# Pair 0 of an attention kernel started from k, q in two halves, constants asked for by GpSimd, zeros multiplied ahead of k

## The chip, the core and the metric

One NeuronCore of a Trainium2 chip runs the whole program. TensorE (PE) multiplies, VectorE (DVE), ScalarE (ACT) and GpSimd (POOL) work element by element, and SyncE (SP) only asks for DMA transfers; ScalarE asks for some too. Each engine takes its instructions in the order written and waits on semaphores. The metric is the device time of one execution in microseconds.

## What is computed

Attention in which a query sees only the keys of its own bucket (six sign bits of a random projection), for 16 heads of 768 rows and 64 columns, and two feed-forward layers behind it:

```python
q_bits = (np.einsum('bhsd,dk->bhsk', q, proj) > 0)
k_bits = (np.einsum('bhsd,dk->bhsk', k, proj) > 0)
mask = q_bucket[:, :, :, None] == k_bucket[:, :, None, :]
scores = scale * np.matmul(q, k.transpose(0, 1, 3, 2))
scores = np.where(mask, scores, -1000000000.0)
attn = np.exp(scores - np.max(scores, axis=-1, keepdims=True))
attn = attn / (np.sum(attn, axis=-1, keepdims=True) + 1e-09)
x = np.matmul(attn, v)
# layer 1: h = x @ w_in, g = P(h) / (Q(h) + 1e-06), x = g @ w_out
# layer 2: h = x @ w_in, g = h - np.tanh(h), out = g @ w_out
```

## The kernel before

Two heads make a pair; there are eight pairs, then the two layers. A pair has 12 tiles of 128 query rows, six of head e=0 and six of head e=1. For each tile TensorE makes scores of 128x768 in one of two PSUM buffers `slot` (`pe_scores`), VectorE takes the row minimum (`dve_rowmin`, L571; scores are negated), ScalarE the exponential E (`act_exp`, L459), TensorE transposes E in two halves into `turn_ps` (`pe_tile`, L379), ScalarE rounds each half to `pt_hi` (L520), VectorE subtracts to get `pt_lo` (L613), and TensorE multiplies both with v (`pe_pv`). Scores are made `AHEAD` = 3 tiles early; `pe_att`, `act_att` and `dve_att` write out the order of each engine tile by tile (n = 0 to 11).

Products keep float32 accuracy by splitting an operand in a rounded high part and the rest. For scores the operands are `opA[e][x]` and `opB[e][x]` (qA, kA, qB, kB in the trace; x = 0 is q, 1 is k). Half of the partitions of opA are "hot" rows, which carry the bucket: q and k are transposed (`turned`, q_t and k_t), multiplied with the projection `proj_bd` (dots), compared with zero (`bits`), the bits multiplied with `pats`, and the result compared with `counts`. A score of two different buckets is then pushed away by 2^120.

While a pair runs, q and k of the next are turned in between its tiles (`pe_turn`, `act_turned`, L266 and L405), and GpSimd splits them. Pair 0 has nobody ahead of it. Its preparation is `pe_first`, `act_first`, `dve_first` and `pool_first`: q is loaded by SP, k by ScalarE, each in two transfers (one for each head). TensorE transposes q in two halves (L296), then k; ScalarE copies q_t and splits q, VectorE copies k_t; four dots give all bits in one tile of 128 partitions, one VectorE instruction makes `bits` (L556), four products the hot rows (L311), which VectorE (q, L563) and ScalarE (k, L431) write. GpSimd makes the low parts of head 0 and then all parts of head 1. Then follow three scores, three row minima (`dve_first` ends with them), and two exponentials (`act_first`). In the first tiles of pair 0 ScalarE also copies the turned q and k of pair 1 (four L405), which wait for GpSimd's count `t_op1`, since `turned` is overwritten.

SP's queue holds, in this order: q, four pieces of the projection, `pats`, `counts`, v, q and k of pair 1 (each waits for the transposes that free its buffer), the coefficients of the layers, six weight tiles, and then what the pairs need.

Of the kernel before, what the change touches and what calls it, by code (L numbers as in the profile page):

```python
# [30 lines left out]
def build(nc, q, k, v, proj, w_in1, w_out1, coef_a, coef_b, w_in2, w_out2,  # L31
# [42 lines left out]
            for names in ADDED_BY.values() for name in names}  # L74
    loads = {name: top.enter_context(nc.semaphore("s_" + name))
             for name in ["ident", "consts", "coefs", "ready", "coef", "proj", "q", "k", "v", "out", "ops0", "ops1",
                          "scale_out0", "scale_out1", "scale_in0", "scale_in1", "shift0", "shift1", "pool_here", "sync_here"]
             + ["t_turn", "t_q", "t_k", "t_dots", "t_bits", "t_hot", "t_hot_q", "t_hot_k",
                "t_hi_q", "t_hi_k", "t_hi_kb", "t_lo", "t_op1"]
# [11 lines left out]
    with top:  # L91
# [70 lines left out]
        first_bank = [[aux_ps, pv_ps], turn_ps]  # L162
        att.close()
# [124 lines left out]

        def pe_first(eng):

            eng.wait_ge(loads["ident"], 16)
            for x in range(2):
                eng.wait_ge(loads["qk"[x]], 32)
                for h in range(2):
                    for c in range(G):
                        mm = eng.transpose(first_bank[x][h][:, c * P:(c + 1) * P],  # L296
                                           nat[x][:, h * G + c, :, :], ident[:, :])
                    mm.then_inc(loads["t_turn"], 1)
            eng.wait_ge(loads["coef"], 1)
            for x in range(2):  # L300
                eng.wait_ge(loads[("t_q", "t_k")[x]], 2)
                for h in range(2):
                    o = (2 * x + h) * KB
                    mm = eng.matmul(slot[0][o:o + KB, 0, 0:HALF], proj_bd[:, x, :],
                                    turned[x][:, h * HALF:(h + 1) * HALF], start=True, stop=True)
            mm.then_inc(loads["t_dots"], 1)
            eng.wait_ge(loads["consts"], 32)
            eng.wait_ge(loads["t_bits"], 1)
            for h in range(2):
                for x in range(2):  # L310
                    eng.matmul(first_bank[x][h][:, 0:HALF], pats[:, 2 * x + h, :], bits[:, :],  # L311
                               start=True, stop=True).then_inc(loads["t_hot"], 1)
# [31 lines left out]
        def pe_att(eng, p, first=False, prepare=True, turn=True, last=False):  # L344
            for n in range(TILES - G * last):
                pe_tile(eng, p, n)
                if first and n < 2:
                    pe_turn(eng, 1, n, 0)
# [8 lines left out]
                if first and n + AHEAD == T:  # L357
                    eng.wait_ge(loads["t_op1"], 6)
# [49 lines left out]

        def act_first(eng):
            hs = [slice(0, HALF), slice(HALF, S)]  # L410
            for h in range(2):
                eng.wait_ge(loads["t_turn"], h + 1)
                eng.activation(turned[0][:, hs[h]], first_bank[0][h][:, 0:HALF], ACT.Copy,
                               scale=-1.0 / float(D) ** 0.5).then_inc(loads["t_q"], 1)
            eng.wait_ge(loads["proj"], 64)
            eng.activation(proj_bd[:, 0, :], proj_bd[:, 0, :], ACT.Copy, scale=-1.0
                           ).then_inc(loads["coef"], 1)
            eng.wait_ge(loads["t_q"], 2)
            eng.activation(opA[0][0][0:D, :], turned[0][0:D, :], ACT.Copy
                           ).then_inc(loads["t_hi_q"], 1)  # L420
            eng.activation(opB[0][0][D:2 * D, :], turned[0][0:D, :], ACT.Copy
                           ).then_inc(loads["t_hi_q"], 1)
            eng.wait_ge(loads["t_k"], 2)
            eng.activation(opA[0][1][0:D, :], turned[1][0:D, :], ACT.Copy
                           ).then_inc(loads["t_hi_k"], 1)
            eng.wait_ge(loads["consts"], 32)
            for e in range(2):
                o = D - e * D
                for h in range(2):
                    eng.wait_ge(loads["t_hot"], 2 * h + 2)  # L430
                    eng.activation(opA[e][1][o:o + D, hs[h]], first_bank[1][h][o:o + D, 0:HALF],  # L431
                                   ACT.Relu, bias=counts[o:o + D, 1:2]
                                   ).then_inc(loads["t_hot_k"], 1)
            eng.wait_ge(loads["ready"], 3)
# [69 lines left out]
        def act_att(eng, p, first=False, prepare=True, turn=True, last=False):  # L504
            for n in range(TILES):
# [17 lines left out]
                if first and n < 2:  # L523
                    eng.wait_ge(loads["t_op1"], 3 * n + 3)
# [21 lines left out]

        def dve_first(eng):
            hs = [slice(0, HALF), slice(HALF, S)]
            for h in range(2):
                eng.wait_ge(loads["t_turn"], h + 3)  # L550
                eng.tensor_copy(turned[1][:, hs[h]], first_bank[1][h][:, 0:HALF]
                                ).then_inc(loads["t_k"], 1)
            eng.wait_ge(loads["t_k"], 2)
            eng.tensor_copy(opB[0][1][0:D, :], turned[1][0:D, :]).then_inc(loads["t_hi_kb"], 1)
# [802 lines left out]
```

## Time and profile before

| | us |
|---|---|
| three runs | 767.23, 767.30, 768.35 (median 767.3) |
| the profiled execution | 767.21 |
| its span, first to last instruction | 765.0 |
| TensorE busy | 751.2 (98%) |
| VectorE, ScalarE, GpSimd busy | 536.6, 478.4, 155.5 |

A row of the timeline tells the start and length of an instruction, or of several of one kind in a row (x2: both together, with what lay between them), and in brackets how long the engine stood idle ahead of it and what ended that. Transfers are listed by the issuing queue (SPq, ACTq); the length there is that of the issue, and landing is told apart. The ends of matmuls are modelled.

### The profile page before, as it was taken

To read this page: it belongs to the slowest core of one execution; us is meant where nothing else is said; L and a number is where in the kernel's file an instruction comes from. 1 tells how busy PE (TensorE), PEld (TensorE's weight loads), DVE (VectorE), ACT (ScalarE), POOL (GpSimd) and SP (SyncE) were. 2 spreads that over 40 slices of the span, in tenths; PEclk is the share of its full clock that TensorE was granted. 3 is DMA by queue.
4 is the path that set the end of the run, shared out by engine and by line. 5 is a ranking of instruction groups with operands and counts; after the bars stand their busy time and mean duration, and the time that the engine had idled before them with its cause. 6 is when DMAs were issued, how large, how long until landed. Compare 5 with 4: busy or idle time off the path is not lost.

```text
span 765.0 us, 11965 instructions
## 1 busy us (share of the span) xinstructions
PE 751.2 (98%) x3840; PEld 642.1 (84%) x3840; DVE 536.6 (70%) x856; ACT 478.4 (63%) x940; POOL 155.5 (20%) x133
## 2 busy tenths in 40 slices
PE   5999999999999999999999999999999999999998
PEld 3899999999998877888888888888888888888886
DVE  4888988988997999999988898955442322233222
ACT  5989988988997877788766876755332222222221
POOL 5784665566566000000000000000000000000000
PEclk9999999999999999999999999999999999999999
DMA  7678778877753410000000233330000100001001
GB/s 196 145 170 204 172 178 185 188 177 179 164 130 99 146 51 32 1 1 1 0 1 15 55 95 99 93 87 1 0 1 1 56 0 1 0 1 56 0 1 56
DMA packets 65243, 58.11 MB, mean 76 GB/s; under 512 B 31792, under 2 KB 50480, under 8 KB 65200
## 3 DMA queue, kind: packets, MB, share of 16 engines
q1 hardware_dynamic: 63488, 57.09, 29.6%
q10 hardware_dynamic: 1712, 0.46, 0.3%
q8 instruction: 25, 0.41, 0.2%
q14 instruction: 18, 0.15, 0.1%
HBM read 29.57 MB, written 3.19 MB: 43 GB/s over the span
## 4 chain that ended last, share of the span: by engine, by line
PE 84%; DVE 12%; issue 2%; ACT 1%; ACTq 0%; DVEq 0%
PE acc L822 28%; PE h_ps L793 27%; PE slot L253 9%; PE turn_ps L379 8%; PE pv_ps L337 4%; PE pv_ps L339 4%; DVE sqr L967 2%; DVE pol L988 2%; DVE pol L999 2%; DVE pol L974 1%; DVE pol L980 1%; PE aux_ps L266 1%; DVE sqr L991 1%; DVE wout_lo L1028 1%; DVE g_lo L1012 1%
## 5 line engine op out<-in xcount | busy, mean ns | idle before, releaser
L793 PE MATMUL h_ps<-x_hi,win_lo 128*128 128x512 f32 x384 | 149.7, 390 | 0.0
L793 PE MATMUL h_ps<-x_lo,win_hi 128*128 128x512 f32 x384 | 149.4, 389 | 0.0
L793 PE MATMUL h_ps<-x_hi,win_hi 128*128 128x512 f32 x384 | 149.4, 389 | 0.0
L843 ACT ACTIVATE g_hi<-pol 128x512 fp32r<-128x512 f32 x96 | 60.8, 633 | 125.6 <-PE acc L822 100.4
L1012 DVE TENSOR_TENSOR g_lo<-pol,g_hi 128x512 fp32r<-128x512 f32 x96 | 66.0, 687 | 97.9 <-ACT g_hi L843 97.7
L613 DVE TENSOR_TENSOR pt_lo<-turn_ps,pt_hi 128x384 fp32r<-128x384 f32 x192 | 97.8, 550 | 18.8 <-ACT pt_hi L520 17.3
L520 ACT ACTIVATE pt_hi<-turn_ps 128x384 fp32r<-128x384 f32 x192 | 84.1, 494 | 15.2 <-PE turn_ps L379 13.8
L571 DVE TENSOR_REDUCE row_min<-slot 128x1 f32<-128x768 f32 x96 | 90.4, 942 | 1.5 <-PE slot L253 1.5
L459 ACT ACTIVATE E<-slot,row_min 128x768 f32<-128x768 f32 x96 | 88.1, 918 | 4.2 <-DVE row_min L571 2.6
L793 PEld LDWEIGHTS h_ps<-x_lo,win_hi 128*128 128x128 f32 x384 | 72.1, 188 | 15.0
L793 PEld LDWEIGHTS h_ps<-x_hi,win_hi 128*128 128x128 f32 x384 | 72.1, 188 | 15.0
L793 PEld LDWEIGHTS h_ps<-x_hi,win_lo 128*128 128x128 f32 x384 | 72.0, 188 | 14.7
L1006 DVE TENSOR_TENSOR pol<-h_ps,mag 128x512 f32<-128x512 f32 x48 | 33.1, 691 | 67.7 <-ACT mag L866 67.2
L379 PE MATMUL turn_ps<-ident,E 128*128 128x128 f32 x576 | 79.6, 273 | 0.0
L866 ACT ACTIVATE mag<-h_ps 128x512 f32<-128x512 f32 x48 | 28.7, 598 | 78.4 <-PE h_ps L793 75.2
L822 PE MATMUL acc<-g_hi,wout_lo 128*128 128x512 f32 x192 | 75.2, 392 | 1.0 <-DVE g_lo L1012 0.8
L822 PE MATMUL acc<-g_hi,wout_hi 128*128 128x512 f32 x192 | 74.7, 389 | 0.0
L822 PE MATMUL acc<-g_lo,wout_hi 128*128 128x512 f32 x192 | 74.7, 389 | 0.0
L822 PE MATMUL acc<-wout_lo,g_hi 128*128 128x512 f32 x192 | 74.7, 389 | 0.0
L822 PE MATMUL acc<-wout_hi,g_hi 128*128 128x512 f32 x192 | 74.7, 389 | 0.0
L822 PE MATMUL acc<-wout_hi,g_lo 128*128 128x512 f32 x192 | 74.7, 389 | 0.0
L379 PEld LDWEIGHTS turn_ps<-ident,E 128*128 128x128 f32 x576 | 68.0, 140 | 5.3 <-DVE pt_lo L613 1.9
(119 smaller groups left out, 1375.6 us busy)
## 6 DMA issues: line engine op xcount, KB each, us to landing
win_raw<-in_moe_w_in SPq DMA_DIRECT2D x32, 256.0 KB, 3.2
wout_raw<-in_moe_w_out SPq DMA_DIRECT2D x32, 256.0 KB, 3.0
q_nat<-in_q SPq DMA_DIRECT2D x16, 192.0 KB, 3.3
v_nat<-in_v SPq DMA_DIRECT2D x8, 384.0 KB, 3.4
scale<-softmax_scale SPq DMA_DIRECT2D x16, 192.0 KB, 3.2
k_nat<-in_k SPq DMA_DIRECT2D x14, 192.0 KB, 3.6
qA<-q_hi SPq DMA_DIRECT2D x14, 192.0 KB, 2.6
qB<-q_hi SPq DMA_DIRECT2D x14, 192.0 KB, 3.0
```

The costliest lines, as they stand in the source:

```text
L253: mm = eng.matmul(slot[m % 2][:, h, 0:HALF], ops[e][0][:, i * P:(i + 1) * P], ops[e][1][:, h * HALF:(h + 1) * HALF], start=first, stop=not ...
L337: eng.matmul(pv_ps[:, 0:HALF], vv, pt_hi[:, c % 2, kt, :], start=kt == 0, stop=False)
L379: mm = eng.transpose(turn_ps[h][:, c3 * P:(c3 + 1) * P], E[:, n % RING, kt * P:(kt + 1) * P], ident[:, :])
L459: eng.activation(halves(E[:, m % RING, :]), slot[m % 2][:, :, 0:HALF], ACT.Exp, bias=row_min[:, m % RING:m % RING + 1], scale=-1.0, accum_ ...
L520: eng.activation(pt_hi[:, c % 2, k0:k0 + T // 2, i * P:(i + 1) * P], turn_ps[h][:, 0:HALF].rearrange("r (k n) -> r k n", n=P), ACT.Copy).t ...
L571: eng.tensor_reduce(row_min[:, m % RING:m % RING + 1], slot[m % 2][:, :, 0:HALF], AX.XY, ALU.min).then_inc(sems["rowmin"], 1)
L613: eng.tensor_tensor(pt_lo[dst], turn_ps[h][:, 0:HALF].rearrange("r (k n) -> r k n", n=P), pt_hi[dst].bitcast(F32), ALU.subtract).then_inc( ...
L793: mm = eng.matmul(h_ps[t % 4][:, :], w[:, ws], columns(x, kt, c), start=kt + n == 0, stop=kt == KT - 1 and n == 2)
L822: mm = eng.matmul(acc[i][:, :], l, r if layer else r[:, :], start=j + n == 0, stop=j == J - 1 and n == 2)
L843: eng.activation(g_hi[:, t % TEMPS, :], pol[:, t % TEMPS, :], ACT.Copy).then_inc(mlp_sems["g_hi"], 1)
L1006: eng.tensor_tensor(pol[:, t % TEMPS, :], h_ps[t % 4][:, :], mag[:, t % 2, :], ALU.subtract).then_inc(mlp_sems["g"], 1)
L1012: eng.tensor_tensor(g_lo[:, b, :], pol[:, b, :], g_hi[:, b, :].bitcast(F32), ALU.subtract).then_inc(mlp_sems["g_lo"], 1)
```

## The change

In pair 0's preparation, and nowhere else:

- **Loads.** SP asks for k of one head, then for q in four pieces (two halves of the rows by two heads); ScalarE asks for the identity and k of the other head. GpSimd asks for `pats`, two pieces of the projection (four before) and `counts`, which SP did.
- **TensorE.** It multiplies zeros (a part of E's last buffer, set by VectorE) ten times, transposes k, then the first half of q. The products of bits and patterns take 32 partitions each. The second half of q is transposed behind k's patterns. Three and four more zero products stand ahead of the first and second scores. The third scores come behind the transposes of tile 0.
- **ScalarE and VectorE.** Each copies one half of k_t. ScalarE makes the projection for q as the negative of that for k, ahead of its copy. Bits are made in three pieces, the low part of q's first half by VectorE (`qB<-q_t,qA`), that of the second half by GpSimd. The row minimum of the third tile is taken behind pt_lo of tile 0.
- **GpSimd.** The casts and subtractions are reordered, k first.
- SP loads q of pair 1 after the transposes of q's second half (`t_turn` 4), k of pair 1 after those of k.

```diff
@@ pe_first
+            eng.wait_ge(loads["ready"], 1)
+            pe_busy(eng, 10)
             eng.wait_ge(loads["ident"], 16)
+            for h in range(2):
+                pe_first_turn(eng, 1, h)
+            pe_first_turn(eng, 0, 0)
+            eng.wait_ge(loads["t_k"], 2)
             eng.wait_ge(loads["coef"], 1)
+            for h in range(2):
+                mm = pe_first_dots(eng, 1, h, slot[1][:, 0, :])
             mm.then_inc(loads["t_dots"], 1)
+            eng.wait_ge(loads["t_q"], 1)
+            pe_first_dots(eng, 0, 0, slot[1][:, 0, :]).then_inc(loads["t_dots"], 1)
...
@@ act_first
+            eng.wait_ge(loads["proj"], 32)
+            eng.activation(proj_bd[:, 0, :], proj_bd[:, 1, :], ACT.Copy, scale=-1.0
+                           ).then_inc(loads["coef"], 1)
+            eng.wait_ge(loads["t_turn"], 2)
+            eng.activation(turned[1][:, HALF:S], first_bank[1][1][:, 0:HALF], ACT.Copy
+                           ).then_inc(loads["t_k"], 1)
+            act_first_q(eng, 0)
             for h in range(2):
+                act_first_hot(eng, 0, h)
+            act_first_q(eng, 1)
+            act_first_hot(eng, 1, 1)
...
@@ dve_first
+            eng.tensor_copy(opA[0][1][0:D, :], turned[1][0:D, :]).then_inc(loads["t_hi_k"], 1)
+            dve_first_bits(eng, slice(2 * KB, 4 * KB), slot[1][:, 0, :], 1)
+            eng.wait_ge(loads["t_hi_q"], 1)
+            eng.tensor_tensor(opB[0][0][0:D, 0:HALF], turned[0][0:D, 0:HALF],
+                              opA[0][0][0:D, 0:HALF].bitcast(F32), ALU.subtract
+                              ).then_inc(loads["t_lo_q"], 1)
+            dve_first_bits(eng, slice(0, KB), slot[1][:, 0, :], 2)
+            dve_first_hot(eng, 0, 0)
...
@@ dve_att
+                if first and n == 0:
+                    dve_rowmin(eng, 0, 2)
...
@@ SP
-                for e in range(2):
-                    eng.dma_start(nat[0][:, :, e, :], q_d[0, :, e]).then_inc(loads["q"], 16)
+                eng.dma_start(nat[1][:, :, 0, :], k_d[0, :, 0]).then_inc(loads["k"], 16)
+                for h in range(2):
+                    tiles = slice(h * G, (h + 1) * G)
+                    for e in range(2):
+                        eng.dma_start(nat[0][:, tiles, e, :], q_d[0, :, e, tiles]
+                                      ).then_inc(loads[("t_q0", "q")[h]], 16)
...
@@ gpsimd
+                eng.dma_start(pats[:, :, :], patterns).then_inc(loads["consts"], 16)
+                eng.wait_ge(loads["ready"], 2)
+                for e in range(2):
+                    eng.dma_start(proj_bd[e * D:(e + 1) * D, 1, e * NB:(e + 1) * NB], proj
+                                  ).then_inc(loads["proj"], 16)
+                eng.dma_start(counts[:, :], bit_counts).then_inc(loads["consts"], 16)
```

VectorE's queue in the preparation, from its copy of k_t to the last hot rows, before (kB0 is opB of head 0; the semaphores it waits for stand in brackets):

```order
L551 COPY k_t<-turn_ps0 128x384 [waits s_t_turn]
L551 COPY k_t<-turn_ps1 128x384 [waits s_t_turn]
L554 CAST kB0<-k_t 64x768 [waits s_t_k]
L556 TENSOR_SCALAR bits<-slot0 128x384 [waits s_t_dots]
L563 TENSOR_SCALAR qA0<-aux_ps,counts 64x384 [waits s_t_hot,s_consts]
L563 TENSOR_SCALAR qA0<-pv_ps,counts 64x384 [waits s_t_hot]
L563 TENSOR_SCALAR qA1<-aux_ps,counts 64x384 [waits s_t_hot]
L563 TENSOR_SCALAR qA1<-pv_ps,counts 64x384 [waits s_t_hot]
```

and after:

```order
L613 COPY k_t<-turn_ps0 128x384 [waits s_t_turn]
L616 CAST kA0<-k_t 64x768 [waits s_t_k]
L599 TENSOR_SCALAR bits<-slot1 64x384 [waits s_t_dots]
L619 TENSOR_TENSOR qB0<-q_t,qA0 64x384 [waits s_t_hi_q]
L599 TENSOR_SCALAR bits<-slot1 32x384 [waits s_t_dots]
L606 TENSOR_SCALAR qA0<-aux_ps,counts 64x384 [waits s_t_hot,s_consts]
L626 TENSOR_SCALAR kA1<-turn_ps0,counts 64x384 [waits s_t_hot]
```

The bits come in pieces, a subtraction of q (L619) stands between the first two, and a hot part of k (L626) is VectorE's now.

The same queue from the first row minimum to that of the fourth tile, before:

```order
L571 TENSOR_REDUCE row_min<-slot0 128x1 [waits s_scores0]
L571 TENSOR_REDUCE row_min<-slot1 128x1 [waits s_scores1]
L571 TENSOR_REDUCE row_min<-slot0 128x1 [waits s_scores0]
L613 TENSOR_TENSOR pt_lo<-turn_ps0,pt_hi 128x3x128 [waits s_pt_hi]
L613 TENSOR_TENSOR pt_lo<-turn_ps1,pt_hi 128x3x128 [waits s_pt_hi]
L571 TENSOR_REDUCE row_min<-slot1 128x1 [waits s_scores1]
```

and after:

```order
L637 TENSOR_REDUCE row_min<-slot0 128x1 [waits s_scores0]
L606 TENSOR_SCALAR qA1<-aux_ps,counts 64x384 [waits s_t_hot,s_consts]
L599 TENSOR_SCALAR bits<-pv_ps 32x384 [waits s_t_dots]
L637 TENSOR_REDUCE row_min<-slot1 128x1 [waits s_scores1]
L606 TENSOR_SCALAR qA0<-pv_ps,counts 64x384 [waits s_t_hot,s_consts]
L606 TENSOR_SCALAR qA1<-pv_ps,counts 64x384 [waits s_t_hot,s_consts]
L679 TENSOR_TENSOR pt_lo<-turn_ps0,pt_hi 128x3x128 [waits s_pt_hi]
L679 TENSOR_TENSOR pt_lo<-turn_ps1,pt_hi 128x3x128 [waits s_pt_hi]
L637 TENSOR_REDUCE row_min<-slot0 128x1 [waits s_scores0]
L637 TENSOR_REDUCE row_min<-slot1 128x1 [waits s_scores1]
```

Two instructions stand between the first and second row minimum, and the third one (slot0) has moved behind the two pt_lo.

GpSimd's queue at its start, before:

```order
L650 TENSOR_TENSOR qB0<-q_t,qA0 64x768 [waits s_t_hi_q]
L650 TENSOR_TENSOR kB0<-k_t,kA0 64x768 [waits s_t_hi_k,s_t_lo]
L660 CAST qA1<-q_t 64x768 [waits s_t_q,s_t_lo]
L662 CAST qB1<-q_t 64x768 [waits s_t_op1]
L664 TENSOR_TENSOR qB1<-q_t,qA1 64x768 [waits s_t_op1]
L660 CAST kA1<-k_t 64x768 [waits s_t_k,s_t_op1]
```

and after:

```order
L1390 DMA pats<-in_patterns 128x512
L1393 DMA proj_bd<-in_proj 64x6 [waits s_ready]
L1393 DMA proj_bd<-in_proj 64x6
L1395 DMA counts<-in_bit_counts 128x2
L727 CAST kB0<-k_t 64x768 [waits s_t_k]
L729 ISA
L729 TENSOR_TENSOR kB0<-k_t,kB0 64x768 [waits s_t_hi_kb]
L719 CAST kA1<-k_t 64x768 [waits s_t_lo]
```

Four transfers stand ahead, and k's parts of head 0 come before all of q's.

## Rows read from the trace of the kernel before

**Rows 1.** The page's first line.

```profile
span 765.0 us, 11965 instructions
```

**Rows 2.** Busy time by stretch: length, engines in order, clock, DMA share, GB/s.

```profile
5.00:10.00 5.00, 4.35 (x20) 2.62 (x20) 1.78 (x3) 3.40 (x6) 1.42 (x1) 1.00 0.96 217
...
25.00:60.00 35.00, 35.00 (x240) 32.78 (x239) 31.05 (x55) 31.43 (x75) 24.50 (x25) 1.00 0.74 169
```

**Rows 3.** Chain of waits, 8 to 26 us: start, length, what.

```profile
18.96 1.01 ACT E L459 x2
...
22.84 0.85 PE aux_ps L275 x8
```

**Rows 4.** Timeline of the issuing queues, 0 to 8 us.

```profile
0.74 1.38 SPq L1203 DMA_DIRECT2D q_nat<-in_q  x2
2.31 2.43 SPq L1210 DMA_DIRECT2D proj_bd<-in_proj  x4
...
1.66 1.44 ACTq L1279 DMA_DIRECT2D k_nat<-in_k  x2
```

**Rows 5.** DMA issues, 0 to 30 us: count, KB each, us to landing.

```profile
proj_bd<-in_proj SPq DMA_DIRECT2D x4, 1.5 KB, 3.8
```

**Rows 6.** Timeline of TensorE, 0 to 26 us.

```profile
5.42 0.88 PE L296 MATMUL aux_ps<-ident,q_nat 128*128 128x128 f32 x3 [5.42 <-DMA q_nat<-in_q]
...
7.16 1.54 PE L296 MATMUL turn_ps<-ident,k_nat 128*128 128x128 f32 x6 [0.23 <-DMA k_nat<-in_k]
...
11.42 0.32 PE L311 MATMUL aux_ps<-bits,pats 128*128 128x384 bf16 x1 [1.23 <-DVE bits L556]
...
13.38 0.59 PE L253 MATMUL slot<-kA,qA 128*128 128x384 f32 x2 [1.15 <-ACT kA L431]
...
17.31 0.82 PE L379 MATMUL turn_ps<-ident,E 128*128 128x128 f32 x6
```

**Rows 7.** Timeline of VectorE, 0 to 26 us.

```profile
9.34 1.47 DVE L554 CAST kB<-k_t 64x768 fp32r<-64x768 f32 x1
10.73 0.54 DVE L556 TENSOR_SCALAR bits<-slot 128x384 bf16<-128x384 f32 x1
11.86 0.62 DVE L563 TENSOR_SCALAR qA<-aux_ps,counts 64x384 fp32r<-64x384 f32 x1 [0.58 <-PE aux_ps L311]
12.40 0.62 DVE L563 TENSOR_SCALAR qA<-pv_ps,counts 64x384 fp32r<-64x384 f32 x1
...
14.35 1.82 DVE L571 TENSOR_REDUCE row_min<-slot 128x1 f32<-128x768 f32 x2 [0.16 <-PE slot L253]
...
18.38 1.01 DVE L613 TENSOR_TENSOR pt_lo<-turn_ps,pt_hi 128x384 fp32r<-128x384 f32 x2
```

**Rows 8.** Timeline of ScalarE, 0 to 26 us.

```profile
6.97 0.49 ACT L413 ACTIVATE q_t<-pv_ps 128x384 f32<-128x384 f32 x1
...
15.39 0.90 ACT L459 ACTIVATE E<-slot,row_min 128x768 f32<-128x768 f32 x1 [1.27 <-issue]
...
16.29 0.89 ACT L459 ACTIVATE E<-slot,row_min 128x768 f32<-128x768 f32 x1
...
17.16 0.20 ACT L438 ACTIVATE cb_abs<-cb 128x2 f32<-128x2 f32 x1
17.83 0.87 ACT L520 ACTIVATE pt_hi<-turn_ps 128x384 fp32r<-128x384 f32 x2 [0.47 <-PE turn_ps L379]
```

**Rows 9.** Timeline of GpSimd, 0 to 26 us.

```profile
8.58 1.82 POOL L650 TENSOR_TENSOR qB<-q_t,qA 64x768 fp32r<-64x768 f32 x1 [8.12 <-ACT qA L419]
...
12.54 0.82 POOL L660 CAST qA<-q_t 64x768 fp32r<-64x768 f32 x1
```

**Rows 10.** Timeline of VectorE and GpSimd near the end of the pairs.

```profile
242.32 1.54 DVE L967 SCALAR_TENSOR_TENSOR sqr<-sqr,cb_abs,mag 128x512 f32<-128x512 f32 x1
...
247.91 0.75 DVE L967 SCALAR_TENSOR_TENSOR sqr<-sqr,cb_abs,mag 128x512 f32<-128x512 f32 x1
...
242.01 1.30 POOL L755 TENSOR_TENSOR win_lo<-win_raw,win_hi 128x512 fp32r<-128x512 f32 x1
```

More of the change, by code:

```diff
@@ L162, in build @@
         first_bank = [[aux_ps, pv_ps], turn_ps]
+        zeros = E[:, RING - 1, 0:HALF // 2].bitcast(BF16)
         att.close()
@@ L287, in pe_hot, with pe_busy, pe_first_turn @@
                        start=True, stop=True).then_inc(sems["aux"], 1)
+        def pe_busy(eng, n):
+            for _ in range(n):
+                eng.matmul(slot[1][:, 1, 0:HALF], zeros[:, 0:P], zeros, start=True, stop=True)
+        def pe_first_turn(eng, x, h):
+            eng.wait_ge(loads[("t_q0", "q", "k", "k")[2 * x + h]], 32)
+            for c in range(G):
+                mm = eng.transpose(first_bank[x][h][:, c * P:(c + 1) * P],
+                                   nat[x][:, h * G + c, :, :], ident[:, :])
+            mm.then_inc(loads["t_turn"], 1)
@@ new lines, in pe_first_dots, with pe_first_hot @@
+        def pe_first_dots(eng, x, h, bank):
+            o = (2 * x + h) * KB
+            return eng.matmul(bank[o:o + KB, 0:HALF], proj_bd[:, x, :],
+                              turned[x][:, h * HALF:(h + 1) * HALF], start=True, stop=True)
+        def pe_first_hot(eng, x, h):
+            rows = slice((2 * x + h) * KB, (2 * x + h + 1) * KB)
+            eng.matmul(first_bank[x][h][:, 0:HALF], pats[rows, 2 * x + h, :], bits[rows, :],
+                       start=True, stop=True).then_inc(loads["t_hot"], 1)
@@ L309, in pe_first @@
             for h in range(2):
-                for x in range(2):
-                    eng.matmul(first_bank[x][h][:, 0:HALF], pats[:, 2 * x + h, :], bits[:, :],
-                               start=True, stop=True).then_inc(loads["t_hot"], 1)
+                pe_first_hot(eng, 1, h)
+            pe_first_turn(eng, 0, 1)
+            eng.wait_ge(loads["t_bits"], 2)
+            pe_first_hot(eng, 0, 0)
+            pe_busy(eng, 3)
             eng.wait_ge(loads["t_hi_q"], 2)
@@ L356, in pe_att @@
                     pe_dots(eng, p + 2)
-                if first and n + AHEAD == T:
-                    eng.wait_ge(loads["t_op1"], 6)
+                if first:
+                    pe_first_operands(eng, n)
                 if n + AHEAD < TILES or not last:
@@ new lines, in dve_first_bits, with dve_first_hot @@
+        def dve_first_bits(eng, rows, bank, n):
+            eng.wait_ge(loads["t_dots"], n)
+            eng.tensor_scalar(bits[rows, :], bank[rows, 0:HALF], 0.0, None, ALU.is_gt
+                              ).then_inc(loads["t_bits"], 1)
+        def dve_first_hot(eng, e, h):
+            o = D - e * D
+            eng.wait_ge(loads["consts"], 32)
+            eng.wait_ge(loads["t_hot"], h + 3)
+            eng.tensor_scalar(opA[e][0][o:o + D, h * HALF:(h + 1) * HALF],
+                              first_bank[0][h][o:o + D, 0:HALF],
+                              counts[o:o + D, 0:1], BIG, ALU.is_lt, ALU.mult
+                              ).then_inc(loads["t_hot_q"], 1)
@@ L618, in dve_att @@
                     dve_scale(eng, p, n // T)
+                if first and n == 0:
+                    dve_rowmin(eng, 0, 2)
                 if last and n == TILES - 3:
@@ L1089, in load_qk @@
                     if is_zero(b - 1):
[L1090 removed]
+                        eng.wait_ge(loads["t_turn"], 4 - 2 * x)
                     else:
@@ L1277, in _ @@
                 eng.dma_start(ident[:, :], identity).then_inc(loads["ident"], 16)
-                for e in range(2):
-                    eng.dma_start(nat[1][:, :, e, :], k_d[0, :, e]).then_inc(loads["k"], 16)
+                eng.dma_start(nat[1][:, :, 1, :], k_d[0, :, 1]).then_inc(loads["k"], 16)
                 eng.preload_act_table_set("natural_log_exp_and_others")
@@ L1292, in _ @@
                 begin(eng, "dve")
+                eng.memset(zeros, 0.0).then_inc(loads["ready"], 1)
                 eng.memset(proj_bd[:, :, :], 0.0).then_inc(loads["ready"], 1)
@@ L1302, in _ @@
                 eng.wait_ge(loads["coefs"], 32)
-                eng.wait_ge(loads["ready"], 2)
+                eng.wait_ge(loads["ready"], 3)
                 dve_att(eng, PAIRS - 1, prepare=False, turn=False, last=True)
```

172 lines of the change are left out of this document (82 added, 90 removed).

## The prediction

> **What bounds the kernel now.** I read the page first, then the busy time by stretch, then the chain of waits, then the first 25 us engine by engine. The span is 765.0 us [rows 1]. From 25 us on TensorE has work all the time: 35.00 of 35.00 us in the stretch 25 to 60 [rows 2], and nothing behind 25 us is touched by the diff. So the change is worth what it moves the point where that regime begins, one for one. The chain of waits shows what sets this point: after the first tiles of pair 0 it runs through ScalarE (E at 18.96, then the copies of q_t and k_t that also turn pair 1) and gets to TensorE at 22.84 [rows 3]. ScalarE's pieces in between follow each other. The number to follow is therefore the start of the third exponential, E of tile 2, at 18.96; I call it E2. Ahead of it stand the first scores at 13.38 (S0) and the first transposes of E at 17.31 [rows 6].
>
> **When k is there.** Let K be the start of the k transposes, now 7.16. Behind q's start at 5.42 TensorE waits for DMA, and 192+64+192 KB have landed (768 rows of 64 floats are 192 KB); at 7.16 all 832 KB [rows 4 to 6]. That is 384 KB in 1.74 us, 221 KB/us. With k asked for first, one half of it from each queue, 192+64+96+192 = 544 KB stand before k's end if transfers are served in the order asked for: K = 5.42 + 96/221 = 5.85. Ends: 5.42, if the first q quarter yields, and 7.16, if the order does not matter. If the patterns (128 KB), now asked for early by GpSimd, go ahead of k too, K is 6.4. I take 5.85, nearest to the two rows it is interpolated from.
>
> **Zeros.** Ten multiplications keep TensorE working from about 1.5. Now six transposes take 1.54 us at 7.16, and six of the same size 0.82 at 17.31 [rows 6]: the slower of the two clock levels (1.2 and 2.4 GHz) by the rate, though the granted clock of that stretch reads 1.00 [rows 2]. I count the k transposes at the fast rate. If the zeros don't raise it, two groups of three and the dot products add about 0.7 us.
>
> **From K to the first scores, new order.** Three transposes reach a reader after 0.52 (17.31 to 17.83), the next three 0.33 later; the copy of 0.49 on ScalarE [rows 8] makes k_t whole at K+1.4. Then GpSimd casts to kB (0.82) and VectorE casts to kA at the same moment. They exclude each other: VectorE's cast of 64x768 at 9.34 took 1.47 us and ended at 10.81, 0.41 behind the end of GpSimd's operation (8.58+1.82 = 10.40) [rows 7, 9]. So GpSimd's low part of k starts at K+1.4+0.82+0.41+0.07 = K+2.7 and ends at K+4.5. Bits of k (0.54), the k patterns and ScalarE's casts all fit beside it. But VectorE's next instruction, the low part of q's first half, reads two operands in SBUF, and such a one waits too: the operation of 242.32 took 1.54 us, with GpSimd busy from 242.01 to 243.31, where its like takes 0.75 at 247.91 [rows 10]. It ended 0.55 behind GpSimd; for 384 columns I take 0.45. VectorE is free at K+4.95. Queued behind it are q's bits (0.54, to K+5.5), the pattern product (0.15+0.44, as from the end of bits at 11.27 over 11.42 to 11.86 [rows 6, 7]), the hot rows (0.62, to K+6.7), and the way to the scores (0.3, as 13.02 to 13.38). S0 = K+7.0 = 12.85, against 13.38: 0.5 us gained out of the 1.3 that k comes earlier. Halving q shortens ScalarE's and VectorE's pieces, but the path now goes through GpSimd.
>
> The Trainium skill (SBUF — State Buffer, Who interferes with whom) states this as a rule: a VectorE instruction with two SBUF inputs and a GpSimd one that reads SBUF lock each other out. It names tensor_tensor, the form used here, where my rows have another form. By its opposite, no lock, the sum would be the fourth rival's below.
>
> **From the first scores to E2.** Now it is 18.96-13.38 = 5.58 us. The first two row minima follow each other (two in 1.82), the exponentials too (15.39, 16.29), and the third row minimum is taken ahead of the first pt_lo at 18.38 [rows 7, 8]. New, on VectorE from S0: first row minimum at 0.97 (13.38 to 14.35), next instruction 0.87 later, then a hot part (0.6) and q's second bits (0.54), so the second row minimum runs from 2.98 to 3.93. It was done at 2.8. ScalarE starts the second exponential at 4.0, and pt_hi stands behind it: 0.87+0.2 for the exponential and the small absolute value (16.29 to 17.36) makes 5.1, where now it is 4.45. pt_lo follows 0.55 later and lasts 0.93 for both halves, and only then comes the third row minimum: 6.57 to 7.5. E2 starts at S0+7.6. The earlier transposes of tile 0 (ahead of the third scores now) don't help, since ScalarE holds them up. That is **2.0 us more** than now, by two things: 1.1 us for the work in between row minima and 0.9 for the row minimum that was moved behind pt_lo.
>
> Sum: E2 = 12.85+7.6 = 20.45 against 18.96, **+1.5 us**. Everything behind it keeps its order on all engines, so the end moves by as much.
>
> **What I cost at nothing.** The three and four zero products: the four (0.66) stand ahead of the second scores, ready at about S0+2.7, and VectorE comes for them at 2.98; if they took 0.3 more they would show. The loads of pair 1: the transposes of q's second half, which they wait for, end at about K+4.0, so q is asked for near 9.9, k behind it, and the second coefficient load is the sixth: 9.9+5x0.61 = 12.9, and with 3.8 us to landing 16.7. ScalarE needs it at S0+4.9 = 17.8 (cover: 1.1 us). The weights are queued behind that, and nobody wants them in this stretch. GpSimd has the same eight pieces of splitting work, one of them half as long, and starts them earlier. SP saves six issues, which nothing waits for.
>
> **GpSimd's four DMAs** have no row. Nearest: SP's issue of the same loads at 0.61 us each (2.43 for four [rows 4]) and 3.8 us to landing [rows 5]. GpSimd has more semaphore additions than ScalarE, which issues its first DMA at 1.22, so I put its first at 1.5, the second projection at 2.7, landed at 6.5. ScalarE wants it at K+0.65 = 6.5, since the negated copy stands before its half of k_t. Just hidden, and no reserve. If an issue costs 0.3 less it is well hidden; if it costs 1.5, it lands at 8.3 and all moves by 1.8. The range keeps both ends, nought and 1.8.
>
> The Trainium skill (DMA: Bandwidth & Descriptors, Latency and other measured facts) gives about 1 us to the first byte for a DMA issued from GpSimd and 0.6 from SP or ScalarE. By that the projection would land at 6.9 and the sum be 1.9; no row here shows it.
>
> **The time.** The profiled execution took 767.21, 2.2 more than its span; the three runs have a median of 767.3, so the two agree to 0.1. 767.21+1.5 = **768.7**. A difference of 0.2%, 1.5 us, is about what can be told from none; my sum is on that edge.
>
> **Rivals.**
> 1. *The transposes of tile 0 decide, not E2* (0.09): the row minimum behind pt_lo would be absorbed further on, since TensorE has more done. Then only the first exponential counts: S0+3.1 = 16.0 (exponential at 2.0, as 13.38 to 15.39, and 1.1 for it and the read behind it, as 15.39 to 16.29 and 0.2) against 17.31, and 767.21-1.3 = 765.9; with the lock missing too, 764.6. Against it: the chain of rows 3 is ScalarE all along, without a gap.
> 2. *GpSimd's loads are late* (0.20). ScalarE's queue stands still for the projection, behind it the copy of k_t, both casts and the bits. It decides from a landing later than 6.5; at 8.3 it gives 770.5. For it: four issues one after the other on an engine that issued none. Against: 24 bytes a row.
> 3. *k isn't earlier* (0.10): transfers share the DMA engines by queue and K stays at 7.16. The same path gives +2.8, 770.0.
> 4. *No lock on the low part of q* (0.12): VectorE would run it at K+3.3 and S0 is K+5.7: 767.4.
> 5. My forecast has the remaining 0.49, within 768.0 (K = 5.42, and smaller pieces) and 769.4 (K = 6.4).
>
> **How the numbers follow.** Faster by over 0.2% (below 765.8): the half of rival 1 that goes with other gains, and what I may have overlooked, 0.08. Slower (above 768.8): rivals 2 and 3, less their small ends, 0.26, and a third of my own case, 0.17: 0.43. The rest, 0.49, is within 0.2%. The range leaves out most of rival 1 and the far end of rival 2: 767.0 to 770.8.
>
> **What would show it.** K near 5.85; VectorE's low part of q at 64x384 lasting over 1 us beside GpSimd's; S0 near 12.9; the third row minimum behind pt_lo, and a ScalarE gap of about a microsecond ahead of E2; E2 near 20.5. I am wrong in the sum if E2 comes before 19, in the method if the end does not move with E2, and rival 2 holds if ScalarE's first operation comes after 6.6.

## Result: 0.44% slower, more than forecast

| | before | after |
|---|---|---|
| median, us | 768.35 (767.17 to 769.79, 9 runs) | 772.17 (770.36 to 773.68, 9 runs) |
| profiled execution | 767.21 | 773.68 |
| its span | 765.0 | 771.9 |

The ratio is 1.0044, 95% interval [1.0032, 1.0057]: 3.4 us (2.5 to 4.4). The forecast was 768.7 with a range that ended at 770.8. Before's own 95 runs beside the experiments lie in groups from 766.8 to 770.5, and the profile that the prediction was read from is one of the fastest group. What parts the groups is taken up at the end of the experiments. So the ratios count below, not the absolute times, and each version has its own runs of before beside it. The profile of after is the slowest of its nine runs, 1.5 us above their median.

I follow K (start of the k transposes), S0 (first scores) and E2 (third exponential). TensorE after, start and length in us, in brackets what ended the idle time:

```profile
span 771.9 us, 12012 instructions
...
1.60 3.38 PE L294 MATMUL slot<-E 128*128 128x384 bf16 x10 [1.60 <-DVE E L1370]
7.45 1.51 PE L299 MATMUL turn_ps<-ident,k_nat 128*128 128x128 f32 x6 [2.47 <-DMA k_nat<-in_k]
...
14.12 1.14 PE L294 MATMUL slot<-E 128*128 128x384 bf16 x3
15.29 0.98 PE L255 MATMUL slot<-kA,qA 128*128 128x384 f32 x2
16.07 0.84 PE L255 MATMUL slot<-kB,qB 128*128 128x384 f32 x2
16.84 1.49 PE L305 MATMUL pv_ps<-q_t,proj_bd 128*32 128x384 f32 x2
18.26 1.46 PE L294 MATMUL slot<-E 128*128 128x384 bf16 x4
19.27 1.09 PE L255 MATMUL slot<-kA,qA 128*128 128x384 f32 x2
20.16 0.63 PE L255 MATMUL slot<-kB,qB 128*128 128x384 f32 x2
...
20.98 0.88 PE L422 MATMUL turn_ps<-ident,E 128*128 128x128 f32 x6
```

These lines answer [rows 6]. K is 7.45, later than before's 7.16. TensorE stood still for 2.47 us behind the zeros. Scores take 0.98 and 0.84 where before had 0.59 for the first pair, and the transposes of k take 1.51 where those of E take 0.88 at 20.98: up to about 20 us TensorE works at the lower of its two levels, the zeros included, and never at the upper one. ScalarE, VectorE and GpSimd in the same stretch, answering [rows 7 to 9]:

```profile
8.11 0.23 ACT L474 ACTIVATE proj_bd<-proj_bd 128x32 f32<-128x32 f32 x1 [4.50 <-DMA proj_bd<-in_proj]
9.00 0.49 ACT L477 ACTIVATE k_t<-turn_ps 128x384 f32<-128x384 f32 x1 [0.66 <-PE turn_ps L299]
...
21.82 0.90 ACT L509 ACTIVATE E<-slot,row_min 128x768 f32<-128x768 f32 x1 [2.84 <-DVE row_min L637]
...
25.23 0.90 ACT L509 ACTIVATE E<-slot,row_min 128x768 f32<-128x768 f32 x1 [1.19 <-DVE row_min L637]
```

```profile
11.68 1.38 DVE L619 TENSOR_TENSOR qB<-q_t,qA 64x384 fp32r<-64x384 f32 x1
...
20.82 0.96 DVE L637 TENSOR_REDUCE row_min<-slot 128x1 f32<-128x768 f32 x1 [1.82 <-PE slot L255]
...
23.31 1.02 DVE L679 TENSOR_TENSOR pt_lo<-turn_ps,pt_hi 128x384 fp32r<-128x384 f32 x2 [0.23 <-ACT pt_hi L570]
24.25 1.81 DVE L637 TENSOR_REDUCE row_min<-slot 128x1 f32<-128x768 f32 x2
```

```profile
2.76 1.05 POOL L1393 DMA_DIRECT2D proj_bd<-in_proj  x2
...
9.56 1.20 POOL L727 CAST kB<-k_t 64x768 fp32r<-64x768 f32 x1 [5.20 <-ACT k_t L477]
10.85 1.80 POOL L729 TENSOR_TENSOR kB<-k_t,kB 64x768 fp32r<-64x768 f32 x1
```

L619 stands locked beside GpSimd's subtraction (1.38 us). The second row minimum waits for TensorE at 20.82, the third one (24.25) comes behind pt_lo, ScalarE waits 1.19 for it, and E2 is 25.23, 6.27 later than before. The span is 6.9 longer, so most of that is there at E2.

The transfers, answering [rows 4, 5]: count, KB each, us from issue to landing.

```profile
q_nat<-in_q SPq DMA_DIRECT2D x4, 96.0 KB, 4.6
...
k_nat<-in_k ACTq DMA_DIRECT2D x1, 192.0 KB, 5.6
pats<-in_patterns POOLq DMA_DIRECT2D x1, 128.0 KB, 4.2
...
proj_bd<-in_proj POOLq DMA_DIRECT2D x2, 1.5 KB, 4.4
```

ScalarE asked for its half of k at 1.67 and got it 5.6 us later, at 7.3; this half sets K. SP's half, asked for at 0.75, took 3.5. No q quarter took more than 4.9, so the second one, asked for near 2.1, had landed by 7.0, ahead of a half of k that was asked for before it.

The regime of [rows 2], in which TensorE always has work, begins later, by its busy time in the stretch 25 to 60 (35.00 of 35.00 before):

```profile
25.00:60.00 35.00, 33.58 (x234) 30.46 (x233) 30.25 (x52) 31.17 (x74) 25.43 (x25) 1.00 0.65 151
```

### The profile page after: what moved, and what is told of

Its sections match the earlier page's. It is cut to its first block, busy times and chain, and to the rows that moved or that the text cites. A ratio compares the mean times of both kernels' runs of the same rounds, so it can differ in the third digit from the quotient of the medians.

```text
span 771.9 us, 12012 instructions
## 1 busy us (share of the span) xinstructions
PE 760.5 (99%) x3857; PEld 645.5 (84%) x3857; DVE 538.0 (70%) x860; ACT 477.8 (62%) x941; POOL 158.3 (21%) x138
## 3 DMA queue, kind: packets, MB, share of 16 engines
HBM read 29.56 MB, written 3.19 MB: 42 GB/s over the span
## 4 chain that ended last, share of the span: by engine, by line
PE 82%; DVE 10%; issue 2%; SPq 1%; ACT 1%; DMA 1%; POOL 0%; DVEq 0%; POOLq 0%; ACTq 0%
PE acc L903 28%; PE h_ps L874 28%; PE slot L255 8%; PE turn_ps L422 7%; PE pv_ps L377 4%; PE pv_ps L379 4%; DVE pol L1069 2%; DVE sqr L1048 1%; DVE pol L1080 1%; DVE pol L1055 1%; PE aux_ps L268 1%; DVE pol L1061 1%; DVE wout_lo L1109 1%; DVE g_lo L1093 1%; DVE sqr L1072 1%
```

## Experiments

Every kernel computes the whole reference. Ratios are to runs of before on the same chip; one hundredth of a per cent is 0.08 us. Two versions compared by their ratios stood mostly on different chips, and where their intervals overlap the text says so. "After" is the changed kernel.

**Zeros left out.** All three groups of zero products removed from after.

```diff
-            pe_busy(eng, 10)
...
-            pe_busy(eng, 3)
...
-            pe_busy(eng, 4)
```

> The changed kernel without any of its zero products (ten, three and four). In its profile TensorE ran at the slower level (384 columns every 0.32 us) until about 20.7 us, so the four zeros stood 1.0 us ahead of the second scores, and the three 1.1 us beside the hot rows. If the zeros cost and don't raise the clock (theory C1): second scores 1.0 us sooner, E of tile 2 near 24.2 instead of 25.23, time 1.0 below the changed kernel's 772.2, so 771.1. If the zeros hold up a clock that would fall further or rise later without them (C2): as slow or slower, 772 to 774, with TensorE slow beyond 20.7. Rival: the zeros are beside other work, no change, 772.2.

Median 771.12 (7 runs), ratio 1.0033 [1.0019, 1.0047], against 1.0044 with them. The zeros bring nothing here. By the medians they cost 1.0, but the intervals overlap, so a cost is not shown. In the profile S0 is 14.77 and E2 23.32, with the second scores at 17.73, right behind the dot products, where after's wait for 1 us of four zeros. TensorE's level was another one too in this profile: it was fast at 11.44 (two pattern products in 0.34, where after's take 0.50) and slow again at the first scores (0.98), behind a gap of 1.10.

**Zeros up to k.** 25 instead of 10.

```diff
-            pe_busy(eng, 10)
+            pe_busy(eng, 25)
```

> The changed kernel with 25 zero products at the start instead of 10, so that TensorE has work from 1.6 us until k is there at 7.4. Theory C (the slower clock level is the largest loss, and it stayed because TensorE stood idle from 5.0 to 7.4): k transposes at 0.11 apart instead of 0.22, first scores at K+7.0 = 14.5 instead of 15.3, E of tile 2 7.6 us behind, near 22.1 instead of 25.2; time 3 us below the changed kernel, 769. Rival (the clock is set by what comes after k, sparse work on TensorE): fast until about 9 and slow again, E of tile 2 near 24.5, time 771.5. Rival (the zeros run over and hold k up): 25 x 0.34 = 8.5 us if the clock never rises, k transposes at 10.1, time 775.

Median 772.67 (4 runs), 1.0056 [1.0034, 1.0079]: no gain, where 769 was expected. TensorE:

```profile
1.60 7.19 PE L294 MATMUL slot<-E 128*128 128x384 bf16 x25 [1.60 <-DVE E L1370]
8.62 0.82 PE L299 MATMUL turn_ps<-ident,k_nat 128*128 128x128 f32 x6
...
15.63 0.98 PE L255 MATMUL slot<-kA,qA 128*128 128x384 f32 x2
```

The engine is fast when k comes (0.82 for six), but the zeros ran at the slow level for most of their time and held k up to 8.62; and the first scores are slow again, behind a wait of 1.74 us for the bits, which stand behind the locked L619 (2.03 us).

**k from one queue.** SP asks for both halves of k ahead of q.

```diff
-                eng.dma_start(nat[1][:, :, 0, :], k_d[0, :, 0]).then_inc(loads["k"], 16)
+                for e in range(2):
+                    eng.dma_start(nat[1][:, :, e, :], k_d[0, :, e]).then_inc(loads["k"], 16)
...
-                eng.dma_start(nat[1][:, :, 1, :], k_d[0, :, 1]).then_inc(loads["k"], 16)
```

> The changed kernel with both halves of k asked for by SP, ahead of q; ScalarE asks for the identity alone. In the changed kernel the half of k in ScalarE's queue was asked for at 1.67 and took 5.6 us to land, that in SP's 3.8. Theory K (ScalarE's queue waits for its share behind SP's): k whole at about 5.2 as q was before, k transposes at 5.4 instead of 7.45, but the projection lands at 7.7 and ScalarE's half of k_t waits for it (8.1), so k_t is whole at 8.6 instead of 9.5: 0.9 us gained, 771.3. If TensorE's clock also rises, since it stands idle for 0.4 us instead of 2.5 (theory C): 2 to 3 us more, 768.5. Rival (transfers come in the order asked for, and k waits for bytes, not for its queue): k lands when it did, 772.2.

Median 770.17 (10 runs), 1.0023 [1.0013, 1.0033]. Its profile:

```profile
5.33 1.25 PE L299 MATMUL turn_ps<-ident,k_nat 128*128 128x128 f32 x6 [0.35 <-DMA k_nat<-in_k]
...
11.71 0.33 PE L310 MATMUL aux_ps<-bits,pats 32*128 32x384 bf16 x1 [1.75 <-DVE bits L599]
...
13.14 0.98 PE L255 MATMUL slot<-kA,qA 128*128 128x384 f32 x2 [0.50 <-ACT kA L468]
```

```profile
9.03 2.04 DVE L619 TENSOR_TENSOR qB<-q_t,qA 64x384 fp32r<-64x384 f32 x1
```

K moves from 7.45 to 5.33, E2 from 25.23 to 22.21, the ratio by 0.21%, 1.6 us (after's profile lies 1.5 above its median, this one 0.5): about so much was lost by asking for k from two queues; the two intervals touch. K holds in every profile of the kind: 5.21 to 5.87 in the six with both halves in SP's queue, 7.10 to 7.77 in the three with two queues that show it. What is left is L619, 2.04 us long here (9.03 to 11.07), and the slow scores behind the gap of 1.75 that it opens.

**Third row minimum back in its old place**, on top of the last one.

```diff
@@ dve_first
+            dve_rowmin(eng, 0, 2)
@@ dve_att
-                if first and n == 0:
-                    dve_rowmin(eng, 0, 2)
```

> Both halves of k asked for by SP, as in the run before, and the row minimum of the third tile put back ahead of pt_lo of tile 0. Theory O (that row minimum is on the path: ScalarE stood idle for 1.2 us ahead of the third exponential): third exponential at 21.1 to 21.3 instead of 22.21, time 1.0 below that kernel's 770.2, so 769.2. Rival (pt_lo of tile 0, 0.9 us later now, holds up the transposes of tile 1 and the gain is given back): 770.2.

Median 769.18 (10 runs), 1.0010 [0.9999, 1.0022]; E2 at 20.78 without a wait of ScalarE, where it was 22.21 with 1.19 of waiting. From the second row minimum to E2 it takes 3.15 instead of 4.41. By the ratios 1.0 us are gained; their intervals overlap, so it is the profiles that show it.

**No lock.** On top of "k from one queue", L619 reads q from PSUM, where it still stands unscaled, and not from q_t.

```diff
-            eng.tensor_tensor(opB[0][0][0:D, 0:HALF], turned[0][0:D, 0:HALF],
-                              opA[0][0][0:D, 0:HALF].bitcast(F32), ALU.subtract
+            eng.scalar_tensor_tensor(out=opB[0][0][0:D, 0:HALF], in0=first_bank[0][0][0:D, 0:HALF],
+                                     scalar=-1.0 / float(D) ** 0.5,
+                                     in1=opA[0][0][0:D, 0:HALF].bitcast(F32), op0=ALU.mult, op1=ALU.subtract
```

> Both halves of k asked for by SP, and VectorE's low part of q's first half reads q from PSUM and not from SBUF (the same numbers: the scale is a power of two), so it has one SBUF input. Theory L (lock): the instruction takes 0.55 instead of 2.04 us, q's bits end at 10.2 and not 11.65, first scores at 11.7 instead of 13.14, third exponential and end 1.4 us sooner: 768.8. If TensorE's shorter gap keeps it at the fast level, 0.5 to 1 more: 768. Rival (the instruction waits for something else, or GpSimd's low part of k, done at 10.66, and what follows set the pace): under 0.5 us gained, 769.8.

Median 767.15 (10 runs), 0.9982 [0.9972, 0.9991], 3.1 us below "k from one queue" by the ratios. VectorE, GpSimd and TensorE in turn:

```profile
8.96 0.55 DVE L619 SCALAR_TENSOR_TENSOR qB<-aux_ps,qA 64x384 fp32r<-64x384 f32 x1
```

```profile
8.78 1.80 POOL L730 TENSOR_TENSOR kB<-k_t,kB 64x768 fp32r<-64x768 f32 x1
```

```profile
11.46 0.59 PE L255 MATMUL slot<-kA,qA 128*128 128x384 f32 x2 [0.51 <-DVE qA L606]
...
13.09 0.82 PE L294 MATMUL slot<-E 128*128 128x384 bf16 x4
13.62 0.64 PE L255 MATMUL slot<-kA,qA 128*128 128x384 f32 x2
```

Beside the same GpSimd operation (8.78 to 10.58) L619 takes 0.55 and not 2.04. That is 1.5. The rest comes from TensorE, whose gap of 1.75 is gone and whose scores stay at 0.59: from S0 to E2 it is 7.60 and not 9.07. In these two profiles one lock cost twice: its own wait, and the level that TensorE lost behind it.

**The same without the queue.** L619 from PSUM on top of after alone.

> The changed kernel with q's low part read from PSUM and nothing else: k still comes over two queues, at about 7.4. By the lock alone 0.8 us are gained (1.38 us becomes 0.55): 771.3 against 772.2. By the lock and TensorE's clock, as with k from SP (3.0 us gained where the lock held 1.5): 770. If the lock does not matter where k is late, since GpSimd is not ahead: 772.2.

Median 769.75 (10 runs), 1.0018 [1.0004, 1.0033], 2.0 us below after. K is 7.77, L619 0.55. TensorE:

```profile
12.54 0.82 PE L299 MATMUL pv_ps<-ident,q_nat 128*128 128x128 f32 x3
13.30 0.33 PE L310 MATMUL aux_ps<-bits,pats 32*128 32x384 bf16 x1
13.56 0.66 PE L294 MATMUL slot<-E 128*128 128x384 bf16 x3
14.73 0.59 PE L255 MATMUL slot<-kA,qA 128*128 128x384 f32 x2 [0.51 <-DVE qA L606]
```

Up to the transposes of 12.54 this is after's profile, 0.3 later. Then it rises to the fast level, where after's stands still for 0.56 us and stays slow until 20. The queue and the lock are separate causes, each with a gain of its own, though this interval just touches after's.

**All three together**: k from one queue, L619 from PSUM, row minimum in its old place.

> Both halves of k asked for by SP, q's low part read from PSUM, and the third row minimum back ahead of pt_lo. If the two savings add (theory: lock and row minimum are separate pieces of one path): third exponential near 18.1 where the kernel with PSUM source had 19.06 and the kernel before 18.96, time 1.0 below 767.15, so 766.2, and faster than the kernel before by 0.2% and more. Rival (with TensorE done sooner something else is last, for instance GpSimd's parts of q for the other head or the coefficient loads): 767.0.

Median 765.91 (765.67 to 768.33, 12 runs), **0.9973 [0.9961, 0.9985]**: 2.1 us faster than before and 5.5 faster than after. Its profile doesn't show the gain over before: it is its second slowest run (767.37), with K at 5.87 and E2 at 18.92, where before has 18.96. Beside it the projection's load was moved from GpSimd to ScalarE:

```diff
@@ scalar
+                eng.wait_ge(loads["ready"], 2)
+                for e in range(2):
+                    eng.dma_start(proj_bd[e * D:(e + 1) * D, 1, e * NB:(e + 1) * NB], proj
+                                  ).then_inc(loads["proj"], 16)
@@ gpsimd
-                eng.wait_ge(loads["ready"], 2)
-                for e in range(2):
-                    eng.dma_start(proj_bd[e * D:(e + 1) * D, 1, e * NB:(e + 1) * NB], proj
-                                  ).then_inc(loads["proj"], 16)
```

> As the run with all three, and the two projection pieces asked for by ScalarE behind the identity and not by GpSimd. With them from GpSimd they were there at 6.8, and ScalarE's half of k_t waited for them until 6.96, though its transposes were done near 6.3. Theory P (projection late): ScalarE's copy of k_t starts near 6.3, third exponential 0.5 sooner than in that run, time 765.7. Rival (the transposes of k at the slow level are done only at 6.7, or the pieces are as late from ScalarE's queue): no gain, 766.2.

Median 766.32 (12 runs), 0.9978 [0.9967, 0.9989]: no gain. The pieces landed 4.3 us after ScalarE's issue, against 3.6 after GpSimd's, and the first operation of ScalarE came at 6.76, where it was 6.98: an earlier request, and almost the same landing. This profile is of a run near the median (765.91, span 764.0), and in it the gain over before is seen, TensorE and ScalarE in turn:

```profile
11.44 0.58 PE L255 MATMUL slot<-kA,qA 128*128 128x384 f32 x2 [0.51 <-DVE qA L606]
```

```profile
17.78 0.90 ACT L509 ACTIVATE E<-slot,row_min 128x768 f32<-128x768 f32 x1
```

E2 is 1.18 earlier than before's, and the span 1.0 shorter.

**All three without zeros.**

> The version with k from SP's queue, the third row minimum early and q read from PSUM (765.9, ratio 0.9973), now without the ten, three and four zero products. If the zeros carry TensorE's clock once nothing holds the preparation up, TensorE falls to the slow level in more of the runs: median 767 or more, a spread of 3 us, first scores at .98+.84 instead of .59+.51, E2 above 20. If the zeros carry nothing there (as when the changed kernel ran without them and gained 1.0), the median stays at 765.9 within 0.4 or falls to 765.5, E2 near 18.5. If transfers decide, K stays at 5.3 to 5.9 and projection, asked for by GpSimd, lands near 6.8 in both cases.

Median 767.56 (766.47 to 768.66, 12 runs), 0.9988 [0.9979, 0.9998]. Here the zeros are worth 0.15%, 1.2 us by the ratios, while in the changed kernel they brought nothing. The intervals overlap a little (0.9979 to 0.9985). In the profile:

```profile
12.26 0.58 PE L255 MATMUL slot<-kA,qA 128*128 128x384 f32 x2 [1.10 <-DVE qA L603]
12.68 0.51 PE L255 MATMUL slot<-kB,qB 128*128 128x384 f32 x2
13.13 1.41 PE L305 MATMUL pv_ps<-q_t,proj_bd 128*32 128x384 f32 x2
14.47 1.01 PE L255 MATMUL slot<-kA,qA 128*128 128x384 f32 x2
```

Without the three zeros TensorE waits 1.10 ahead of the first scores and falls to the slow level just behind them (1.41 for two dots, 1.01 for the second scores). With them the wait is 0.50 and the like rows read 0.83 and 0.64.

**Is it the clock in before, too?** Twelve zeros ahead of q in before, then also five behind the dot products, five ahead of the first scores and six ahead of the third; and before unchanged, for a second profile.

```diff
@@ pe_first, in before
+            eng.wait_ge(loads["ready"], 1)
+            for _ in range(12):
+                eng.matmul(slot[1][:, 1, 0:HALF], zeros[:, 0:P], zeros, start=True, stop=True)
...
+            for _ in range(6):
+                eng.matmul(pv_ps[:, 0:HALF], zeros[:, 0:P], zeros, start=True, stop=True)
```

> The kernel before with twelve zero products on TensorE ahead of q's transposes and nothing else (VectorE sets the zeros). In its profile TensorE started at 5.42 and ran slow until about 9.3. Theory C: fast from about 5.4, k transposes 0.33 and k_t 0.7 us sooner, first scores 0.3 to 0.7 us sooner, time 766.6 to 767.1 against 767.3 of undisturbed runs. Rival (the clock's rise and fall does not follow from zeros ahead, or falls again in the gaps at 10.2 to 11.4 and 14.9 to 16.5): scores slow in the first tiles, up to 3 us more, 770. Rival (other engines set the pace): no change.

> The kernel before with twelve zero products ahead of q's transposes, five between dots and hot rows, five ahead of the first scores and six ahead of the third, in banks that nobody uses then. The runs of the kernel before lie in groups: 767.1 to 767.5 at a mean clock of 1.000, 767.7 to 768.4 at 0.998, 769 at 0.996, and some at 770. Theory C (these groups are TensorE slow in more or less of the first 20 us, by what it did in its gaps): the upper groups go, runs between 766.9 and 767.6, median 767.3 against 768.7. Rival (the groups have nothing to do with the gaps): the same spread, median 768.7. Rival (zeros at the slow level overrun the gaps): more runs at 770 and above.

> The kernel before, unchanged, for a second profile of it. If the run falls in one of the slower groups (two in three do), theory C expects TensorE's matmuls at twice the length somewhere between 9 and 20 us, and the third exponential later than 18.96 by what the run is longer; the rival (the difference arises later in the kernel) expects it at 18.96.

The zeros at the start alone change nothing: 1.0007 [0.9992, 1.0022], 10 runs from 767.09 to 769.98. In their profile the k transposes take 0.97 and not 1.54, yet E2 is 18.92: other engines set the pace there. With the gaps filled, the median is 767.40, 0.9985 [0.9974, 0.9995], and 11 runs lie between 766.89 and 767.64, while before's 27 on the same chip go from 767.0 to 770.36. The fastest run with zeros is only 0.1 faster than before's fastest; what the zeros do is take away everything above 767.7. The second profile of before (769.15, span 767.0) shows what such a run is. Busy time by stretch, with the granted clock in the third column from the right:

```profile
10.00:15.00 5.00, 3.09 (x16) 1.78 (x11) 3.87 (x7) 2.35 (x5) 4.71 (x5) 0.91 0.90 219
15.00:20.00 5.00, 4.06 (x16) 3.49 (x15) 2.88 (x4) 2.64 (x7) 4.61 (x4) 0.50 0.59 199
```

and on its TensorE

```profile
16.99 0.98 PE L253 MATMUL slot<-kA,qA 128*128 128x384 f32 x2 [0.94 <-ACT E L459]
17.77 0.84 PE L253 MATMUL slot<-kB,qB 128*128 128x384 f32 x2
18.41 1.48 PE L379 MATMUL turn_ps<-ident,E 128*128 128x128 f32 x6
```

From 15 to 20 us the granted clock is 0.50, 1.2 instead of 2.4 GHz; the transposes of tile 0 take 1.48 where [rows 6] have 0.82, and E2 is 21.00 and not 18.96. That is 2.04 of E2 for 2.0 of the span: the same program as in [rows 6].

Each run also has a granted clock averaged over its span, and by it before's 95 runs fall apart: from 766.8 to 767.7 us it reads 0.999 or 1.000 (35 runs), from 767.5 to 768.7 it reads 0.997 or 0.998 (19), from 768.8 to 769.6 it reads 0.996 (24). So the slower of these three groups are those in which TensorE was granted less of its clock. The 17 runs above 769.7 break the order: 16 of them read 1.000 again. By my reading they are runs in which TensorE doesn't rise at all in the start, since after's profile, slow until 20, reads 1.00 as well; no profile fell in that group.

## Why the prediction was wrong, step by step

**The measure held.** Differences of the span against before's, with those of E2 in brackets: after 6.9 (6.3), k from one queue 3.7 (3.3), no lock 0.8 (0.1), row minimum back 2.2 (1.8), all three 0.4 (0.0), projection by ScalarE -1.0 (-1.2), before again 2.0 (2.0). The end moves with E2 within 0.7 us in all profiles. What the rest of up to 0.7 is, I haven't traced. With it rival 1 falls (the transposes of tile 0 decide and the later row minimum is absorbed): putting that row minimum back moved E2 and the end together.

E2 was forecast at 20.45 and came at 25.23 in a profile that lies 1.5 above after's median. The 4.8 us fall on three terms; in a run at the median they are smaller together, and no profile tells which of them is:

1. **When k is there: +1.6.** K = 5.85 assumed that transfers are served in the order asked for. That step failed across the two queues. This is rival 3 (K stays at 7.16), to which I gave 0.10. "k from one queue" shows it: with both halves at the head of SP's queue K is 5.33, even under the 5.42 that I had as the lower end (over the six profiles with k in one queue it is 5.21 to 5.87). The Trainium skill (DMA: Bandwidth & Descriptors, Issuing engines are not separate DMA queues) says that transfers of different issuers run on the same DMA engines and interleave. The late landing of ScalarE's half, 5.6 us against 3.5 for SP's, fits it.
2. **Zeros, "I count the k transposes at the fast rate": +0.84 from K to S0** (7.84 against 7.0). Of this 0.64 is there when k_t is whole, at K+2.04 and not K+1.4: the 0.7 that I had named as the other end. The order of events behind it was right: GpSimd's cast was held by VectorE's (1.20), its low part followed, L619 was locked until 0.41 behind GpSimd's end (I took 0.45). Rival 4, no lock, falls. The Trainium skill (SBUF — State Buffer, Who interferes with whom) states the rule for an instruction with two SBUF inputs, and that one with at most one, outside the modes that use both ports, doesn't contend; the rows bear out both halves, 1.38 and 2.04 us against 0.55.
3. **From S0 to E2: +2.3** (9.94 against 7.6). The order was right, the rate wasn't. All of it lies ahead of the second row minimum, which starts at S0+5.53. In "no lock", where TensorE is fast from S0 on, it starts at S0+3.19 (14.65, the second scores at 13.62), and S0 to E2 is 19.06-11.46 = 7.60, the forecast figure. "The same without the queue" gives both figures again (3.19, and 22.33-14.73 = 7.60). So the slow level adds 2.34: to the first scores, to the dot products (1.49 for 0.83), to the zeros (1.46 for 0.82) and to the second scores. The step that failed stands under what I cost at nothing: "the four (0.66)" with 0.3 us to spare. I had priced the slow level for the transposes of k and the dots (0.7) and for nothing behind S0. At the slow level nothing is to spare, and TensorE, not VectorE, sets the second row minimum: VectorE waits 1.82 for it.

The 0.9 for the row minimum moved behind pt_lo was about right: putting it back gave 1.0 by the ratios, and 1.26 between the second row minimum and E2 in the profiles.

**GpSimd's loads (rival 2)** were late: the second piece was asked for at 3.3 and not 2.7 and took up to 4.8 us, not 3.8. The transfers of `proj_bd` in after:

```profile
DMA to landing us min/median/max: 4.0/4.4/4.8
```

ScalarE's first operation came at 8.11, close to that rival's 8.3. It cost nothing here, because k came late as well: the copy of k_t at 9.00 waited for TensorE. With K at 5.33 it shows: ScalarE starts at 6.9 there, though the transposes end at 6.58, and k_t is whole at 7.50, K+2.2.

**The baseline.** I argued from three runs with a median of 767.3 and one profile at the fast level. Before's later runs have medians of 767.7 to 769.0. This was bad luck: the profile and two of three runs fell in the fastest group. Of the 3.5 us by which after's median missed the forecast, 1.1 is this (768.35 for 767.3) and 2.4 the slowdown beyond the 1.4 that I had.

**What stays open** is what decides in a given run whether TensorE gets and keeps its fast level. Falls in the profiles came behind gaps of 1.10 to 1.75 us, but [rows 6] have gaps of 1.23 and 1.15 and no fall, and before with zeros at the start has one of 1.68 and none:

```profile
11.37 0.32 PE L315 MATMUL aux_ps<-bits,pats 128*128 128x384 bf16 x1 [1.68 <-DVE bits L560]
```

In after's profile there is no fall at all: TensorE had work from 7.45 on with no gap over 0.56 and rose only near 20. That the lock's gap is what kept it down is argued from one profile with the lock and one without ("the same without the queue"), not shown.

## What to carry to other kernels

Where two queues feed one consumer at the start, don't count on the order of the requests across them; put what is needed first at the head of one queue. Filling TensorE with zeros brought nothing while a stall opened gaps behind them (1.0044 with, 1.0033 without), and 0.15% once it was gone: first take out the stall (here an instruction with two SBUF operands beside GpSimd, mended by reading one operand from PSUM), then fill. In a start that is bound by latency, price TensorE's pieces at both rates, and take the spread of the kernel before as a sign that both occur.

## What the runs showed of the hardware

- The granted clock in the profile doesn't tell the level at the start. After reads 1.00 in every stretch up to 25 us, while its scores take 0.98 instead of 0.59:

```profile
15.00:20.00 5.00, 4.97 (x13) 2.56 (x13) 2.60 (x4) 1.59 (x4) 4.71 (x5) 1.00 1.07 241
```

  Compare this with 0.50 in the same stretch of "before again", at the same rates. In the profiles here the column fell only where TensorE had been fast before. The length of a known instruction is the surer sign.
- Ten zero products of 384 columns take 3.38 us, so they run at the slow level themselves. With a gap of 2.47 us behind them the transposes of k were as slow (1.51) as without any zeros (1.51 in "zeros left out"). The gap's length doesn't order the rest: six took 1.51 behind 0.23 us ("no lock"), 0.99 behind 0.31, 1.25 behind 0.35, 1.04 behind 0.52 and 1.51 again behind 0.89 ("all three").
- The small loads of the projection were slow to land whoever asked: 1.5 KB took 3.3 to 4.9 us in the first 8 us. The Trainium skill (DMA: Bandwidth & Descriptors, Latency and other measured facts) gives about 1 us to the first byte from GpSimd; these rows hold the whole landing, beside 960 KB of q, k, identity and patterns, and leave that figure open.
